# A routed two-layer product over 43 token tiles: hidden products made one tile ahead instead of two

## The chip, the core and the metric

The kernel runs on one core of a Trainium2 chip. The metric is device time in microseconds (us) for one execution. The engines are called as the profile calls them: PE (TensorE, with its weight loads as PEld), DVE (VectorE), ACT (ScalarE), POOL (GpSimd) and SP (SyncE).

## The reference

Three computations follow one another. The last of them, a mixture of experts with one expert for each token, is the part that this study is about.

```python
x = attention(q, k, v)                      # 8 x 576 tokens, 512 wide, linear attention
x = soft_mixture(x, phi, w1, w2)            # 32 slots; each token is a mixture of 32 slot outputs
# the last part, N = 4608 tokens, E = 8 experts, F = 1024
e_idx = np.argmax(x @ w_gate, axis=1)
gate_w = softmax(x @ w_gate)[arange(N), e_idx]
eom = 1 / (1 + exp(-(x @ w_output_gate)))
for e in range(E):
    mask = e_idx == e
    h = np.maximum(x[mask] @ w1[e], 0.0)
    out[mask] = gate_w[mask, None] * eom[mask, e, None] * (h @ w2[e])
```

## The kernel before

The first 318 us of the execution compute the attention, the slots, the gates, and a split of every expert's second weight into a high and a low float16 part (`w_pair`); the first weight is multiplied with the 32 slot outputs beforehand (`g_pair`). The tokens are sorted by expert into tiles of 128 rows. Room is made for `TILES` = 43 tiles, the most that 8 experts can need. In this execution tokens fill 36 of them, which PE's 864 long products (line 1773, 24 a tile) show; tiles 36 to 42 are empty.

Then comes the tile stage, a pipeline over the 43 tiles with two buffers of each kind (n = tile modulo 2):

- POOL **gathers** the sorted rows of a tile from a table in HBM by an indirect DMA (line 571), and later **stores** the result rows by an indirect DMA (line 578). Both stand in one queue; the order is written out by hand.
- DVE's `take` (line 1308) copies the gathered row into `c_rows`.
- PE's `turn` (line 1755) transposes it into bank 7, and DVE's `turn` (line 1312) copies it out to `c_stack`, counted by `cs_copied`. There is one such bank, so PE's next `turn` waits for DVE's last.
- PE's `hidden` (line 1761) makes 8 products of 128 columns into two banks, after reading the tile's expert number into a register (line 1759).
- ACT's `relu` (line 894, two halves) writes the high part `h_hi`; DVE's `low` (line 1318, two halves) writes the low part `h_lo`.
- PE's `second` (line 1773) makes 24 products of 512 columns into bank 4 + n, after another read of the expert number (line 1768). DVE's `finish` (line 1326) scales that into `y_out`, and POOL stores it.

PE makes `hidden` of tile t+2 just before `second` of tile t, in `step`. DVE's step t is turn(t+3), take(t+4), low(t+1), finish(t). From tile 36 on, PE runs `last_step`: it reads from `ended` whether tile t is empty, and if it is, skips both `hidden(t + 2)` and `second(t)`; two products of 2 by 2 (lines 1811 and 1813) stand in for them and raise the counts `y_done` and `h_done`. ACT, DVE and POOL run all 43 tiles in full; an empty tile's rows have row numbers out of bounds, so its gathers and stores move nothing.

## Time and profile before

| what | value |
|---|---|
| median of three executions | 567.01 us (564.3 to 567.61) |
| the profiled execution | 564.3 us, span 562.4 us |
| tile stage, from the first `take` to the last store's issue | 319.07 to 554.14 us |
| PE busy | 425.7 us, 76% of the span |
| DVE busy | 316.6 us, 56% |
| ACT busy, POOL busy | 222.4 us, 228.1 us |
| mean granted TensorE clock | 0.906 |

The clock is given as a share of 2.4 GHz; 0.50 is 1.2 GHz. The execution's own time is 1.9 us more than its span. Times inside the trace count from the span's start. A line number with a trailing "q" at its engine (PEldq, DVEq) is an instruction of that engine's sequencer, which reads the program and hands work to the engine.

### The profile page before, as it was taken

The numbers are of one execution on the slowest core, as the hardware profiler recorded it, in microseconds if no ns is written. First come the engines' busy times: TensorE is split into PE (matmuls) and PEld (weight loads), VectorE is DVE, ScalarE is ACT, GpSimd is POOL, SyncE is SP. The second block draws the span as 40 slices with busy tenths as digits, with TensorE's granted clock in tenths as the row PEclk, the third lists the DMA queues.
The fourth block names the chain that finished last, engine by engine and source line by source line (L and its number), as shares of the span: only waits on it lengthen the run. The fifth ranks groups of instructions, "written<-read, shape, count | busy, mean of one in ns | idle before, by whom it ended". The sixth has DMA issues, their size and how long they took to land.

```text
span 562.4 us, 12505 instructions
## 1 busy us (share of the span) xinstructions
PE 425.7 (76%) x4517; PEld 250.4 (45%) x4518; DVE 316.6 (56%) x491; ACT 222.4 (40%) x328; POOL 228.1 (41%) x145
## 2 busy tenths in 40 slices
PE   0468898888786627456677389999999999999910
PEld 0456676666454324352223144545454545454400
DVE  5999999994156460378396633434343433434372
ACT  0366676667313869484724211212121212121140
POOL 2255555553010487975500223333424242433342
PEclk9999999999769868677799679999999999999965
DMA  9769999956399999999595001111111111111100
GB/s 302 251 216 383 366 388 378 386 189 226 116 337 375 341 395 368 378 369 327 219 355 206 5 4 61 40 59 40 58 41 58 41 58 41 54 45 44 49 20 2
DMA packets 44855, 106.75 MB, mean 190 GB/s; under 512 B 4560, under 2 KB 5648, under 8 KB 44816
## 3 DMA queue, kind: packets, MB, share of 16 engines
q1 hardware_dynamic: 37888, 95.42, 46.1%
q0 software_dynamic: 4816, 10.06, 5.6%
q10 hardware_dynamic: 2112, 0.71, 0.6%
q8 instruction: 30, 0.49, 0.4%
q14 instruction: 9, 0.07, 0.0%
HBM read 96.25 MB, written 11.88 MB: 192 GB/s over the span
## 4 chain that ended last, share of the span: by engine, by line
PE 50%; DVE 16%; DMA 13%; ACT 7%; issue 6%; POOL 5%; SPq 0%; DVEq 0%; POOLq 0%; ACTq 0%
PE banks L1773 33%; DMA ring<-in_moe_w 6%; DMA big<-in_moe_w 4%; PE banks L1761 3%; DVE big L936 3%; POOL big L525 2%; DVE big L909 2%; PE banks L1638 2%; POOL big L554 2%; ACT big L712 2%; PE banks L1387 2%; DVE big L922 2%; PE banks L1558 1%; DVE big L928 1%; PE banks L1583 1%
## 5 line engine op out<-in xcount | busy, mean ns | idle before, releaser
L1773 PE MATMUL banks<-big,work 128*128 x864 | 193.8, 381 | 0.5 <-issue 0.5
L1773 PEld LDWEIGHTS banks<-big,work 128*128 128x128 f16 x864 | 83.4, 98 | 95.2 <-issue 2.5
L894 ACT ACTIVATE work<-banks 128x512 f16<-128x512 f32 x86 | 46.6, 595 | 185.7 <-PE banks L1773 170.4
L1326 DVE TENSOR_SCALAR work<-banks,tok,unscale 128x512 f32<-128x512 f32 x43 | 34.8, 809 | 130.2 <-PE banks L1773 124.9
L578 POOL DMA_INDIRECT out<-work,token_of x43 | 43.6, 1013 | 136.7 <-DVE split_ct L1308 124.4
L571 POOL DMA_INDIRECT tok<-token_rows,token_of x43 | 44.0, 1023 | 40.9 <-DVE token_of L1210 25.4
L525 POOL TENSOR_TENSOR big<-big 128x1152 f32<-128x1152 f32 x16 | 33.6, 2118 | 58.9 <-DVE big L941 58.9
L1318 DVE SCALAR_TENSOR_TENSOR work<-banks,work 128x512 f16<-128x512 f32 x86 | 55.0, 680 | 0.0
L1387 PE MATMUL banks<-big 64*64 64x128 f32 x1152 | 37.5, 283 | 7.5 <-ACT big L605 6.1
L1387 PEld LDWEIGHTS banks<-big 64*64 64x64 f32 x1152 | 33.8, 140 | 13.7 <-ACT big L605 11.7
L909 DVE TENSOR_REDUCE big<-big 128x256 f32<-128x2304 f32 x8 | 34.1, 4266 | 6.9 <-DMA big<-in_k 6.9
L518 POOL TENSOR_TENSOR big<-big 128x2304 f32<-128x2304 f32 x8 | 32.4, 4054 | 10.5 <-DVE big L928 10.4
L554 POOL TENSOR_TENSOR big<-big 128x2048 f16<-128x2048 f32 x8 | 32.6, 4079 | 8.7 <-ACT big L719 8.7
L554 POOL TENSOR_TENSOR big<-kvg,big 128x2048 f16<-128x2048 f32 x4 | 16.3, 4083 | 34.6 <-ACT kvg L719 34.6
L1761 PE MATMUL banks<-split_ct,kvg 128*128 128x128 f16 x304 | 24.9, 224 | 3.2 <-issue 1.9
L1638 PE MATMUL banks<-ring,split_ct 128*32 128x512 f32 x128 | 18.5, 704 | 10.4 <-ACT work L788 5.4
L1077 DVE TENSOR_REDUCE top_all<-banks 128x1 f32<-128x257 f32 (+1 forms) x16 | 5.7, 356 | 35.7 <-PE banks L1602 23.8
L605 ACT ACTIVATE big<-big 128x1152 f32<-128x1152 f32 x16 | 18.5, 1154 | 17.8 <-DVE big L922 17.7
L1421 PE MATMUL banks<-ident,big 128*128 128x128 f32 x144 | 21.9, 285 | 4.6 <-ACT kvg L663 3.7
L1558 PE MATMUL banks<-big,slot_in 128*32 128x256 f32 x192 | 15.6, 465 | 12.8 <-ACT side L730 7.2
L1072 DVE TENSOR_REDUCE top<-big 128x1 f32<-128x2048 f32 x8 | 18.1, 2276 | 9.3 <-DMA big<-in_moe_w 9.3
L1761 PEld LDWEIGHTS banks<-split_ct,kvg 128*128 x304 | 19.6, 98 | 8.4 <-issue 3.8
(219 smaller groups left out, 646.9 us busy)
## 6 DMA issues: line engine op xcount, KB each, us to landing
ring<-in_moe_w SPq DMA_DIRECT2D x12, 2048.0 KB, 10.2
big<-in_moe_w SPq DMA_DIRECT2D x10, 2048.0 KB, 11.6
big<-in_k SPq DMA_DIRECT2D x8, 1152.0 KB, 6.3
big<-in_q SPq DMA_DIRECT2D x8, 1152.0 KB, 7.0
big<-in_v SPq DMA_DIRECT2D x8, 1152.0 KB, 9.3
big<-in_moe_w SPq DMA_DIRECT2D x8, 1024.0 KB, 10.0
kvg<-in_moe_w SPq DMA_DIRECT2D x4, 1024.0 KB, 8.3
ring<-in_moe_w SPq DMA_DIRECT2D x4, 1024.0 KB, 10.7
```

What stands on the lines that cost most here:

```text
L518: pool.tensor_tensor(q_view(Q[b % 2]), q_view(Q[b % 2]), over_d(qtop[:, b % 2, :]), ALU.subtract).then_inc(q_shifted, 1)
L525: pool.tensor_tensor(q_view(QE[b % 3][:, part]), q_view(QE[b % 3][:, part]), over_d(qstat[:, b % 2, rec]), ALU.mult).then_inc(q_normed, 1)
L554: pool.tensor_tensor(lo, raw[:, u * HALF:(u + 1) * HALF], hi, ALU.subtract).then_inc(w_split, 1)
L571: pool.indirect_dma_start(out=srt[:, t, :], out_offset=None, in_=table, in_offset=bass.IndirectOffsetOnAxis(ap=token_of[:, t:t + 1].bitcas ...
L578: pool.indirect_dma_start(out=out, out_offset=bass.IndirectOffsetOnAxis(ap=token_of[:, t:t + 1].bitcast(U32), axis=0), in_=y_out[n], in_of ...
L894: act.activation(h_hi[n][:, b * 512:(b + 1) * 512], psum[2 * n + b], ACT.Relu).then_inc(h_hi_ready, 1)
L909: dve.tensor_reduce(out=kmax, in_=blocks(K[b % 2]).rearrange("p h (c d) -> p h d c", c=C), axis=X, op=ALU.max).then_inc(kmax_done, 1)
L1318: dve.scalar_tensor_tensor(h_lo[n][:, part], psum[2 * n + b], 0.0, h_hi[n][:, part], ALU.max, ALU.subtract).then_inc(h_lo_ready, 1)
L1326: dve.tensor_scalar(y_out[n], psum[4 + n], srt[:, ds(t, 1), NS], unscale[:, ds(ev, 1)], ALU.mult, ALU.mult).then_inc(y_scaled, 1)
L1387: last = pe.matmul(psum[a][64 * h:64 * h + 64, g * P:(g + 1) * P], blocks(K[b % 2])[r, 2 * g + h, c * D:(c + 1) * D], v_and_ones, start=c ...
L1761: i = pe.matmul(psum[2 * n + j // 4][:, j % 4 * P:(j % 4 + 1) * P], g_pair[:, ds(ev, 1), j * P:(j + 1) * P].rearrange("p o f -> p (o f)"), ...
L1773: last = pe.matmul(psum[4 + n], h[n][:, j * P:(j + 1) * P], w_pair[:, ds(ev, 1), w, j, :].rearrange("p o n -> p (o n)"), start=j == 0 and ...
```

## The change

The hidden products are made one tile ahead instead of two. PE's start-up loses one `turn` and one `hidden`; PE's step t becomes turn(t+2), hidden(t+1), second(t). DVE's step t becomes turn(t+2), take(t+3), low(t+1), finish(t). POOL starts with 5 gathers instead of 6, and gathers tile t+5 instead of t+6 after storing tile t. The separate `last_step` is gone: for the tiles from 36 on, `hidden(t+1)` is made whether or not a tile is empty, and only `second` stands under the condition. In `hidden` the read of the expert number stands before the wait for `cs_copied`. In `second` the waits for `h_hi` and `h_lo` are split: for the first half before product 0, for the second half before product 12. ACT's program is the same.

```diff
-            for t in range(2, 6):
+            for t in range(2, 5):
                 pool.wait_ge(c_rows_ready, t - 1)
                 gather(t)
             for t in range(TILES):
                 store(t, t % 2)
-                if t + 6 < TILES:
-                    pool.wait_ge(c_rows_ready, t + 5)
-                    gather(t + 6)
+                if t + 5 < TILES:
+                    pool.wait_ge(c_rows_ready, t + 4)
+                    gather(t + 5)
...
             take(2, 0, 32)
+            low(0, 0)
             turn(1, 1)
-            take(3, 1, 32)
-            low(0, 0)
-            turn(2, 0)
 
             def step(t, n, stored, count, static=None):
                 m = 1 - n
+                if static is None or static + 2 <= TILES - 1:
+                    turn(t + 2, n)
                 if static is None or static + 3 <= TILES - 1:
-                    turn(t + 3, m)
-                if static is None or static + 4 <= TILES - 1:
-                    take(t + 4, n, count)
+                    take(t + 3, m, count)
...
-            def hidden(t, n, early=True):
-
+            def hidden(t, n):
                 ev = pe.value_load(tile_e[0:1, ds(t, 1)], min_val=0, max_val=E - 1)
+                pe.wait_ge(cs_copied, t + 1)
...
-            def second(t, n, reused):
+            def second(t, n, reused, surely=True):
                 ev = pe.value_load(tile_e[0:1, ds(t, 1)], min_val=0, max_val=E - 1)
                 if reused:
                     pe.wait_ge(y_scaled, t - 1)
...
+                products_ = [(j, m) for j in range(FC) for m in range(3)]
+                if surely:
+                    for j, m in products_:
+                        if j % 4 == 0 and m == 0:
+                            pe.wait_ge(h_hi_ready, 2 * t + (j // 4 + 1))
+                            pe.wait_ge(h_lo_ready, 2 * t + (j // 4 + 1))
+                        last = products(j, m)
+                else:
+                    pe.wait_ge(h_hi_ready, 2 * t + 2)
+                    pe.wait_ge(h_lo_ready, 2 * t + 2)
+                    over = pe.value_load(ended[0:1, ds(t, 1)], min_val=0, max_val=E)
+                    with pe.If(over < E):
+                        for j, m in products_:
+                            products(j, m)
+
+                    last = pe.matmul(psum[6][0:2, 0:2], ones16[:, :], ones16[:, :], start=True, stop=True)
+                last.then_inc(y_done, 1)
...
-            hidden(1, 1)
-            turn(2, 0)
-
-            def step(t, n, static=None):
-                turn(t + 3, 1 - n)
-                pe.wait_ge(cs_copied, t + 3)
-                pe.wait_ge(h_hi_ready, 2 * t + 2)
-                pe.wait_ge(h_lo_ready, 2 * t + 2)
-                hidden(t + 2, n)
-                second(t, n, static is None).then_inc(y_done, 1)
...
+            def step(t, n, static=None, surely=True):
+                if static is None or static + 2 <= TILES - 1:
+                    turn(t + 2, n)
+                if static is None or static + 1 <= TILES - 1:
+                    hidden(t + 1, 1 - n)
+                second(t, n, static != 0 and static != 1, surely)
```

On DVE, at the start of the tile stage (`split_ct<-tok` is take, `split_ct<-banks` is turn, `work<-banks,work` is low), the two programs differ so:

```order
 L1312 COPY split_ct<-banks 128x128 [waits cs_done]
 L1308 COPY split_ct<-tok 128x128 [waits gathered0]
-L1312 COPY split_ct<-banks 128x128 [waits cs_done]
+L1318 SCALAR_TENSOR_TENSOR work<-banks,work 128x512 [waits h_hi_ready] x2
+L1312 COPY split_ct<-banks 128x128 [waits cs_done] x2
 L1308 COPY split_ct<-tok 128x128 [waits gathered1]
 L1318 SCALAR_TENSOR_TENSOR work<-banks,work 128x512 [waits h_hi_ready] x2
-L1312 COPY split_ct<-banks 128x128 [waits cs_done] x2
```

The first `low` stands one `turn` and one `take` earlier, ahead of the `take` of tile 3.

On PE, at the head of a step in the loop, the program before has the end of `second`, then `turn`, then `hidden` (`banks<-split_ct,kvg`):

```order
619 L1773 MATMUL banks<-big,work 128x512 x2
620 L1752 REGISTER_ALU
621 L1755 MATMUL banks<-ident,split_ct 128x128 [waits cs_copied,c_rows_ready]
622 L1792 ISA [waits cs_copied]
623 L1759 ISA [waits h_lo_ready,h_hi_ready]
624 L1759 TENSOR_LOAD tile_e
625 L1759 ISA x2
626 L1761 ISA
627 L1761 MATMUL banks<-split_ct,kvg 128x128
```

The waits for `h_lo` and `h_hi` stood ahead of the read of the expert number and of `hidden`.

The changed program has there, on PE:

```order
601 L1772 MATMUL banks<-big,work 128x512 x2
602 L1750 REGISTER_ALU
603 L1753 MATMUL banks<-ident,split_ct 128x128 [waits cs_copied,c_rows_ready]
604 L1756 ISA
605 L1756 TENSOR_LOAD tile_e
606 L1756 ISA x2
607 L1759 ISA [waits cs_copied]
608 L1759 MATMUL banks<-split_ct,kvg 128x128
```

Only the wait for `cs_copied` is left ahead of `hidden`, and it stands behind the read.

The waits for `h_lo` and `h_hi` now stand ahead of `second` on PE:

```order
622 L1759 MATMUL banks<-split_ct,kvg 128x128
623 L1766 TENSOR_LOAD tile_e
624 L1766 ISA x2
625 L1780 ISA [waits y_scaled]
626 L1772 ISA [waits h_lo_ready,h_hi_ready]
627 L1772 MATMUL banks<-big,work 128x512
```

They moved past `hidden` and past the second read of the expert number.

In a step of the tiles from 36 on, PE had this before (`<-side` is the read of `ended`):

```order
682 L1755 MATMUL banks<-ident,split_ct 128x128 [waits cs_copied]
683 L1804 ISA [waits cs_copied]
684 L1806 ISA [waits h_lo_ready,h_hi_ready]
685 L1806 TENSOR_LOAD side
686 L1806 ISA x2
687 L1807 COMPARE_AND_BRANCH
688 L1759 ISA
```

The branch stood ahead of `hidden`, so an empty tile cost one read.

The changed program has there, behind its 8 `hidden` products:

```order
684 L1766 ISA
685 L1766 TENSOR_LOAD tile_e
686 L1766 ISA x2
687 L1768 REGISTER_ALU
688 L1784 ISA [waits y_scaled]
689 L1786 REGISTER_ALU [waits h_lo_ready,h_hi_ready]
690 L1786 TENSOR_LOAD side
691 L1786 ISA x2
692 L1787 COMPARE_AND_BRANCH
```

The branch stands behind `hidden` and behind a read of the expert number.

On POOL, at the last stores and gathers of the program (`tok<-` is a gather, `out<-` a store):

```order
 L578 DMA out<-work,token_of 4608x512 [waits y_scaled]
 L571 DMA tok<-token_rows,token_of 128x33 [waits c_rows_ready]
-L578 DMA out<-work,token_of 4608x512 [waits y_scaled] x6
+L578 DMA out<-work,token_of 4608x512 [waits y_scaled]
+L571 DMA tok<-token_rows,token_of 128x33 [waits c_rows_ready]
+L578 DMA out<-work,token_of 4608x512 [waits y_scaled] x5
 L51 UNCONDITIONAL_BRANCH
```

The last gather stands behind one more store.

## Rows read from the trace of the kernel before

**Rows 1.** The chain that ended last, in order of time: start us, us, what.

```profile
327.99 6.80 PE banks L1773 x24
...
340.53 0.45 PE banks L1761 x8
340.98 5.18 PE banks L1773 x24
346.21 0.45 PE banks L1761 x8
```

**Rows 2.** Busy time of each engine in the middle stretch, granted clock, DMA.

```profile
340.00:530.00 190.00, 190.00 (x1109) 95.46 (x1107) 75.61 (x170) 36.90 (x68) 67.43 (x67) 1.00 0.15 48
```

**Rows 3.** PE's sequencer, 340.5 to 346.2: operation, ns min/median/max, first and last start us.

```profile
L1793 PEldq EVENT_SEMAPHORE  x1: 51/51/51, 342.9 to 342.9; - x1
...
L1759 PEldq TENSOR_LOAD <-tile_e x1: 300/300/300, 343.1 to 343.1; - x1
...
L1768 PEldq TENSOR_LOAD <-tile_e x1: 300/300/300, 344.9 to 344.9; - x1
L1768 PEldq SEQ_ASSERT  x1: 18/18/18, 345.6 to 345.6; - x1
```

**Rows 4.** Timeline, one step: start us, us, engine, line, operation [idle before].

```profile
341.58 1.28 DVE L1318 SCALAR_TENSOR_TENSOR work<-banks,work 128x512 f16<-128x512 f32 x2
```

**Rows 5.** Timeline of the first tiles.

```profile
322.48 0.20 DVE L1308 COPY split_ct<-tok 128x128 f16<-128x128 f16 x1 [2.54 <-DMA tok<-token_rows,token_of]
...
323.85 1.28 DVE L1318 SCALAR_TENSOR_TENSOR work<-banks,work 128x512 f16<-128x512 f32 x2
...
325.05 0.21 DVE L1312 COPY split_ct<-banks 128x128 f16<-128x128 f16 x1
...
326.28 1.19 PE L1761 MATMUL banks<-split_ct,kvg 128*128 128x128 f16 x8 [0.61 <-issue]
...
327.99 6.80 PE L1773 MATMUL banks<-big,work 128*128 x24 [0.52 <-issue]
```

**Rows 6.** PE's sequencer before the first long product, 325 to 328.2.

```profile
L1754 PEldq EVENT_SEMAPHORE  x1: 51/51/51, 325.3 to 325.3; - x1
...
L1768 PEldq TENSOR_LOAD <-tile_e x1: 306/306/306, 327.2 to 327.2; - x1
```

**Rows 7.** Half a microsecond in which the clock rises: us, PE busy, PEclk.

```profile
330.50:331.00 0.50, 0.50 (x3) 0.54 0.00 0
```

**Rows 8.** Timeline of the empty tiles.

```profile
536.84 1.02 POOL L571 DMA_INDIRECT tok<-token_rows,token_of  x1 [0.31 <-issue]
...
538.17 1.02 POOL L578 DMA_INDIRECT out<-work,token_of  x1 [0.30 <-issue]
539.49 1.02 POOL L571 DMA_INDIRECT tok<-token_rows,token_of  x1 [0.31 <-issue]
540.37 0.20 DVE L1308 COPY split_ct<-tok 128x128 f16 x1 [3.42 <-DMA tok<-token_rows,token_of]
...
540.70 0.29 PE L1755 MATMUL banks<-ident,split_ct 128*128 128x128 f16 x1 [3.10 <-DVE split_ct L1308]
...
542.56 0.18 DVE L1308 COPY split_ct<-tok 128x128 f16<-128x128 f16 x1
...
543.34 1.02 POOL L578 DMA_INDIRECT out<-work,token_of  x1 [2.82 <-DVE work L1326]
...
544.70 1.28 DVE L1318 SCALAR_TENSOR_TENSOR work<-banks,work 128x512 f16<-128x512 f32 x2
...
547.05 0.16 PE L1811 MATMUL banks<-ones 128*2 128x2 f16 x1 [1.73 <-ACT work L894]
...
549.41 0.98 POOL L578 DMA_INDIRECT out<-work,token_of  x1 [0.93 <-DVE work L1326]
...
552.53 0.81 DVE L1326 TENSOR_SCALAR work<-banks,tok,unscale 128x512 f32<-128x512 f32 x1 [1.95 <-DMA out<-work,token_of]
554.14 0.98 POOL L578 DMA_INDIRECT out<-work,token_of  x1 [1.77 <-DVE work L1326]
```

More of the change, by code:

```diff
@@ L1346, in step @@
                 finish(t, n, stored)
-            step(0, 0, None, 48, 0)
+            step(0, 0, None, 32, 0)
             step(1, 1, None, 48, 1)
-            with dve.Fori(1, (TILES - 5) // 2) as h:
-                step(2 * h, 0, h, 16 * h + 48)
+            with dve.Fori(1, (TILES - 5) // 2 + 1) as h:
+                step(2 * h, 0, h, 16 * h + 32)
                 step(2 * h + 1, 1, h, 16 * h + 48)
-            for t in range(TILES - 5, TILES):
-                step(t, t % 2, t // 2, 16 * ((t + 4) // 2 + 1), t)
+            for t in range(TILES - 3, TILES):
+                step(t, t % 2, t // 2, 16 * ((t + 3) // 2 + 1), t)
         @block.tensor
@@ L1770, in second, with products @@
                     pe.wait_ge(y_scaled, t - 1)
-                for j in range(FC):
-                    for m, (h, w) in enumerate(((h_hi, 0), (h_hi, 1), (h_lo, 0))):
-                        last = pe.matmul(psum[4 + n], h[n][:, j * P:(j + 1) * P],
-                                         w_pair[:, ds(ev, 1), w, j, :].rearrange("p o n -> p (o n)"),
-                                         start=j == 0 and m == 0, stop=j == FC - 1 and m == 2)
-                return last
+                def products(j, m):
+                    h, w = ((h_hi, 0), (h_hi, 1), (h_lo, 0))[m]
+                    return pe.matmul(psum[4 + n], h[n][:, j * P:(j + 1) * P],
+                                     w_pair[:, ds(ev, 1), w, j, :].rearrange("p o n -> p (o n)"),
+                                     start=j == 0 and m == 0, stop=j == FC - 1 and m == 2)
+                products_ = [(j, m) for j in range(FC) for m in range(3)]
[14 more added lines that the diff above has]
+                last.then_inc(y_done, 1)
             pe.wait_ge(g_split, E)
@@ L1781, in _ @@
             turn(0, 0, False)
-            pe.wait_ge(cs_copied, 1)
             hidden(0, 0)
             turn(1, 1)
-            pe.wait_ge(cs_copied, 2)
-            hidden(1, 1)
-            turn(2, 0)
-            def step(t, n, static=None):
-                turn(t + 3, 1 - n)
-                pe.wait_ge(cs_copied, t + 3)
-                pe.wait_ge(h_hi_ready, 2 * t + 2)
-                pe.wait_ge(h_lo_ready, 2 * t + 2)
-                hidden(t + 2, n)
-                second(t, n, static is None).then_inc(y_done, 1)
-            def last_step(t, n, static=None):
-                if static is None or static + 3 <= TILES - 1:
-                    turn(t + 3, 1 - n)
-                follows = static is None or static + 2 <= TILES - 1
-                if follows:
-                    pe.wait_ge(cs_copied, t + 3)
-                pe.wait_ge(h_hi_ready, 2 * t + 2)
-                pe.wait_ge(h_lo_ready, 2 * t + 2)
-                over = pe.value_load(ended[0:1, ds(t, 1)], min_val=0, max_val=E)
-                with pe.If(over < E):
-                    if follows:
-                        hidden(t + 2, n, False)
-                    second(t, n, True)
-                pe.matmul(psum[6][0:2, 0:2], ones16[:, :], ones16[:, :], start=True, stop=True).then_inc(y_done, 1)
-                if follows:
-                    pe.matmul(psum[6][0:2, 0:2], ones16[:, :], ones16[:, :], start=True, stop=True).then_inc(h_done, 2)
+            def step(t, n, static=None, surely=True):
[4 more added lines that the diff above has]
+                second(t, n, static != 0 and static != 1, surely)
             step(0, 0, 0)
```

8 lines of the change are left out of this document (4 added, 4 removed).

## The prediction

> **What bounds the kernel now.** I read the chain that ended last first, because the change touches one stage only and the page's shares are averages over many. The reader is to see in it a step of 5.68 us: hidden products start at 340.53 us and again at 346.21, 0.45 us of them, then 24 long products of 5.18 us, and nothing between [rows 1]. The row by stretches says the same: PE is busy 190.00 of 190.00 us at a granted clock of 1.00 [rows 2]. So in tiles 1 to 35 PE's array is the bound, and a change of order can win nothing there; it can only open gaps. The stage has two ends where PE is not full, the start (until the first long product at 327.99 us) and the empty tiles (from about 533.6 us: 327.99 + 6.80 + 35 x 5.68). There other waits end last, and there the change is decided. Next I read PE's sequencer rows, which tell how far the sequencer runs ahead of the array, and the two timelines.
>
> **Full tiles: nothing.** The products per tile are the same, and between the first long product and the last the array still has 35 groups of hidden products. DVE's turn, take, low and finish keep their order, and gather t+5 behind store t is taken in DVE's step t+2, as gather t+6 was. What is new is cover: hidden(t+1) comes 5 us before its tile's second, not 11 us. But relu waited until the buffer's last user, second(t-1), was done in both programs, so it starts only the 0.45 us of the hidden products later. Low runs from 341.58 to 342.86 [rows 4]; allow 0.5 us, 343.4. The long products that need it start about 346.66 on the array. Cover is left: 3.3 us. The sequencer comes earlier. Before, it stood at the wait for low until 342.9, read the expert number at 343.1, again at 344.9, and was past that read at 345.6 [rows 3], 1 us before the array wanted the long products. With the wait moved behind the hidden products, it passes from turn straight to the read, some 0.6 us sooner, and finds low done. The four added or moved semaphore waits cost about 0.05 us each (the duration of such an instruction in rows 3) on a sequencer that is 1 us ahead: I take 0. The bounds: below, 0, since the array has no gap to give; above, four fully exposed ones, 0.2 us a step, 7 us in 35.
>
> **The start: a gain of 1.2 us.** Before, the first long product hung on take(3) and turn(2): low(0) at 323.85, the copy of tile 2 at 325.05, hidden products at 326.28, long ones at 327.99 [rows 5]. Now low(0) stands right behind take(2), which started at 322.48 and takes 0.20 us; low(0) begins at 322.68 and the copy of tile 1 follows it after the same 1.20 us, at 323.88 instead of 325.05. PE has the same to do behind it: turn, read, 8 hidden products, read, long products. In the trace that took 327.99 - 325.05 = 2.94 us, so the first long product starts at 326.8, 1.2 us earlier. hidden(0) may start 0.3 to 0.5 us sooner by its earlier read; low(0) waits for the gather of tile 2 anyway, so this is covered. What the clock does with the 1.2 us is a bound. It rose from 1.2 to 2.4 GHz near 330.95 [rows 7], some 3 us into the first group, which took 6.80 us instead of 5.18. If it rises with the work, all 1.2 us stay. If it rises at the same instant, the 1.2 us are run at half speed and 0.6 stay. If it rises clearly sooner, up to 1.6 us more come (the whole excess of 6.80 over 5.18). I take 1.2, since the pattern of work ahead of it is the same but for one group of eight products.
>
> Here a page speaks. In the row, the sequencer stood at the wait for `cs_copied` of line 1754 until 325.3, just after the copy ended, and only then went on to its read [rows 6]. The Trainium skill, "Perfetto Trace Analysis", section "Sequencer Loop", has it that an engine instruction is pushed into a queue and waits for its semaphores there, so the sequencer goes on. By that rule the read would be done while turn waits, and the start would gain 2.0 us, not 1.2. The row shows the wait as an instruction of the sequencer's own, so I keep 1.2 and price the other below as a rival.
>
> **The empty tiles: a loss of 4.6 us.** Two prices change.
>
> First, the gather. Before, tile 42 was gathered behind store(36), at 539.49, and taken at 542.56 without a wait; that is 3.07 us at most. The gather at 536.84, behind a store with real data, was taken at 540.37, 3.53 us later. Now tile 42 is gathered behind store(37), which starts at 543.34; a gather follows a store by 1.32 us (538.17 to 539.49), so at 544.66, and take(42) comes at 547.7 (548.2 by the other row). Before, DVE had begun low(40) at 544.70 [rows 8]. That alone is 3.1 us.
>
> Second, PE's sequencer. An empty tile before cost turn, one read of `ended`, a branch and two tiny products: low ended at 544.70 + 1.28 = 545.98 and the tiny product started at 547.05, 1.07 us [rows 8]. Now each empty tile up to 41 has a read of the expert number, 8 hidden products, a second read, and only then that 1.07. A read until its first product is 327.99 - 327.2 = 0.79 us [rows 5, 6]; the pushing of 8 products is 327.2 - 326.28 = 0.92. So 0.79 + 0.92 + 0.79 + 1.07 = 3.57 us a step, where a step took some 2.0 us before. Followed through:
> - take(40) is still released at 540.37 by the gather behind store(35), and PE's turn at 540.70; the tiny product of step 38 starts at 544.3, of step 39 at 547.9.
> - turn(42) needs take(42) at 547.7 plus 0.33, so 548.0: the two prices meet here, and do not add. Step 40 ends at 551.6, step 41 at 555.2.
> - step 42 has no hidden products: 0.79 + 1.07, so 557.1. DVE's last finish follows at once; before it was at 552.53.
> - its other condition, the output buffer: finish(40) 551.7, its store 1.61 us behind (552.53 to 554.14), free 3.12 us after that (549.41 to 552.53), so 556.4. Not the later one.
>
> The loss is 557.1 - 552.5 = 4.6 us. What follows the last finish, the store at 554.14 and the end of the program, only shifts. Finish(37) is not moved, since PE's step 37 ends near 538.5 (533.6, some 1.3 us for DVE's finish and take, and 3.57), and DVE comes to it at 541.7 after the late gather. Bounds: 3.1 if only the gather counts and DVE keeps its old pace; 5.9 if the gather takes 3.53 and the hidden products at the low clock (1.19 us instead of 0.92, [rows 5]) are exposed three times.
>
> **Sum.** 0 - 1.2 + 4.6 = +3.4 us. On the profiled execution that is 564.3 to 567.7. That one is the fastest of the three runs; the median, 567.01, is 2.7 us above it, and the same sum on it gives **570.4 us**.
>
> **Rivals.**
> - *The program does more than is written for the start* (the sequencer does go on past a waiting turn). Then hidden products follow the copy's end, 324.1, by 0.2 us, and the long ones follow at 324.3 + 0.92 + 0.79 = 326.0. A gain of 2.0, so 569.6. For it: an earlier read is what the edit in `hidden` makes possible. Against it: rows 6. Chance 0.10.
> - *The tail is covered.* The reads overlap with the waits, the gather of empty rows lands within 0.5 us, and only the start counts: 565.8. Against it: the take at 540.37 waited 3.42 us for a gather of empty rows. Chance 0.07.
> - *Slower by more than 1%: the full tiles open a gap.* The place is the head of `second`: if the sequencer is not ahead when it comes to the moved waits, the reads and waits show on the array, as they did at the start, where the array stood 0.61 us ahead of the hidden and 0.52 us ahead of the long products [rows 5]. Four exposed waits give +7, so 577; both gaps whole would give 1.13 x 35 = 40 us, 610. It decides from (5.7 - 3.4) / 35 = 0.07 us a step. Against it: the lead of 1 us in rows 3, which grows. Chance 0.08, nearly all at the small end.
> - *The clock stays low through the first tile*, since one group of hidden products less precedes it. The 17 long products after the rise would cost 0.21 us more each, +3.6, so 574. Chance 0.05.
> - *Faster by more than 1%* needs a shorter step, and the array has none to give, so a tail shorter than before. Chance 0.02.
>
> **How the numbers follow.** My forecast has the remaining 0.68, with its own range from 567 to 573. A measurement of this kernel can tell about 1% (5.7 us) from no change. Slower by over 1%: the two slow rivals, 0.13, and the upper end of my tail, 0.04, so 0.17. Faster: 0.02. Same: 0.81. Range: the sum's lowest is 3.1 - 2.8 = +0.3 and its highest 5.9 - 0.6 = +5.3, so 567.3 to 572.3; the runs shown lie 0.6 above and 2.7 below their median, and the covered tail at 565.8 lies just under it. I take 566.0 to 573.3.
>
> **What would show it.** The step stays 5.68 us and PE busy 190 of 190 in the middle. The first long product starts at 326.8. The take of the last tile waits about 3 us for its gather. The tiny products of the last tiles lie 3.6 us apart instead of 2, and the last finish is 4.6 us later with respect to the end of the last long product. It is wrong if gaps stand ahead of the first or the thirteenth long product of a tile, or if the first group takes far more than 6.8 us.

## The result, and the profile after

The changed kernel takes 569.84 us (median, 566.71 to 571.44) against 565.91 us (564.3 to 567.8) of the kernel before in the same series, 14 runs each: a ratio of 1.0062, with a 95% interval of 1.0043 to 1.0083. It is slower by 3.9 us, less than 1%. Its profiled execution took 569.95 us, its span is 568.2 us.

The two profiled executions differ by 5.8 us in their spans, but 2.0 us of that lie ahead of the changed stage: the first take starts at 321.04 us instead of 319.07, in code that the change does not touch. From here on the stage is measured from its own marks: the first take, the first long product, and DVE's finish of tiles 0, 35 and 42 (all from the timelines).

| stretch, us | before | after | difference |
|---|---|---|---|
| first take to first long product | 8.92 | 7.67 | -1.25 |
| first long product to finish(0) | 6.95 | 7.68 | +0.73 |
| finish(0) to finish(35), 35 full tiles | 198.93 | 198.93 | 0.00 |
| finish(35) to finish(42), the empty tiles | 18.66 | 22.97 | +4.31 |
| sum | 233.46 | 237.25 | +3.79 |

**The full tiles.** The chain that ended last in the changed kernel, in order of time (start us, us, what; line 1772 is the long products, 1759 the hidden ones):

```profile
341.97 0.45 PE banks L1759 x8
342.42 5.18 PE banks L1772 x24
...
347.65 0.45 PE banks L1759 x8
```

The period is 347.65 - 341.97 = 5.68 us, as in [rows 1], and the row by stretches (us, PE, PEld, DVE, ACT, POOL, clock, DMA) has PE full, as in [rows 2]:

```profile
340.00:530.00 190.00, 190.00 (x1109) 95.46 (x1108) 74.25 (x166) 35.99 (x67) 67.91 (x67) 1.00 0.15 49
```

PE's sequencer in one of these steps (ns min/median/max, first and last start us). The long products of this step start at 342.42:

```profile
L1756 PEldq TENSOR_LOAD <-tile_e x1: 303/303/303, 338.3 to 338.3; - x1
...
L1766 PEldq TENSOR_LOAD <-tile_e x1: 305/305/305, 340.1 to 340.1; - x1
L1766 PEldq SEQ_ASSERT  x1: 18/18/18, 340.7 to 340.7; - x1
```

The read for the hidden products is at 338.3 and the read for the long ones over at 340.7, 1.7 us ahead of the array, where it was 1 us before [rows 3]. Low for the next tile is done early too:

```profile
343.02 1.28 DVE L1318 SCALAR_TENSOR_TENSOR work<-banks,work 128x512 f16<-128x512 f32 x2
```

It ends at 344.30, and the long products that need it start at 347.65 + 0.45 = 348.10, so 3.8 us of cover are left in this step.

**The start.** The timeline of the changed kernel, to be held against [rows 5]:

```profile
324.46 0.20 DVE L1308 COPY split_ct<-tok 128x128 f16<-128x128 f16 x1 [2.55 <-DMA tok<-token_rows,token_of]
324.57 1.28 DVE L1318 SCALAR_TENSOR_TENSOR work<-banks,work 128x512 f16<-128x512 f32 x2
...
325.77 0.22 DVE L1312 COPY split_ct<-banks 128x128 f16<-128x128 f16 x1
...
326.91 1.16 PE L1759 MATMUL banks<-split_ct,kvg 128*128 128x128 f16 x8 [0.51 <-DVE split_ct L1312]
...
328.71 7.53 PE L1772 MATMUL banks<-big,work 128*128 x24 [0.64 <-ACT work L894]
```

low(0) follows take(2) directly, and the first long product starts 4.25 us after take(2) instead of 5.51. From the copy of tile 1 (325.77) to the first long product it is 2.94 us, as it was from the copy of tile 2 before. But its group takes 7.53 us, where it took 6.80. Half microseconds of the same stretch (us, PE busy, PEclk, DMA share, GB/s):

```profile
330.50:331.00 0.50, 0.50 (x3) 0.50 0.00 0
...
333.00:333.50 0.50, 0.50 (x4) 0.85 0.00 0
```

The clock is still 0.50 (1.2 GHz) at 331 and rises to 2.4 GHz within the row at 333.0, some 4.4 us after the first long product; before it was 3 us after [rows 7]. That takes 0.7 of the 1.25 us back. Counted from the first take, the rise comes after 12.1 us here and after 11.9 us before: work that started earlier did not bring it forward.

**The empty tiles.** The timeline of the changed kernel, to be held against [rows 8] (line 1791 is the tiny product, 1308 take, 571 the gather, 1326 finish):

```profile
540.28 0.16 PE L1791 MATMUL banks<-ones 128*2 128x2 f16 x1 [1.76 <-issue]
540.60 0.20 DVE L1308 COPY split_ct<-tok 128x128 f16 x1 [2.14 <-DMA tok<-token_rows,token_of]
...
543.51 0.20 DVE L1308 COPY split_ct<-tok 128x128 f16 x1 [0.64 <-DMA tok<-token_rows,token_of]
...
544.91 1.02 POOL L571 DMA_INDIRECT tok<-token_rows,token_of  x1 [0.31 <-issue]
...
544.97 0.16 PE L1791 MATMUL banks<-ones 128*2 128x2 f16 x1 [1.88 <-DVE work L1318]
...
547.23 0.20 DVE L1308 COPY split_ct<-tok 128x128 f16 x1 [0.95 <-DMA tok<-token_rows,token_of]
...
548.95 0.16 PE L1791 MATMUL banks<-ones 128*2 128x2 f16 x1 [1.65 <-DVE work L1318]
...
552.78 0.16 PE L1791 MATMUL banks<-ones 128*2 128x2 f16 x1 [1.47 <-DVE work L1318]
...
556.19 0.17 PE L1791 MATMUL banks<-ones 128*2 128x2 f16 x1 [1.44 <-DVE work L1318]
...
557.98 0.16 PE L1791 MATMUL banks<-ones 128*2 128x2 f16 x1 [1.63 <-DVE work L1326]
...
558.29 0.81 DVE L1326 TENSOR_SCALAR work<-banks,tok,unscale 128x512 f32<-128x512 f32 x1 [0.98 <-PE banks L1791]
```

The tiny products lie 4.69, 3.98, 3.83, 3.41 and 1.79 us apart. Tile 42 is taken at 547.23, 2.32 us after its gather was issued and after 0.95 us of waiting; the next tiny product, at 548.95, is not late by it. So in this run it is not the gathers that set the pace. Nor is it low. Low of tile 40 and the sequencer's wait for it (line 1785, in `second` of tile 40, whose tiny product is the one at 552.78):

```profile
547.55 1.29 DVE L1318 SCALAR_TENSOR_TENSOR work<-banks,work 128x512 f16<-128x512 f32 x2
```

```profile
L1785 PEldq EVENT_SEMAPHORE  x1: 51/51/51, 551.7 to 551.7; - x1
```

Low ends at 548.84, and the sequencer comes to the wait 2.9 us later.

The take that the gather behind store(35) releases came 2.32 us after that gather here (538.28 to 540.60) and 3.53 us after it in the kernel before (536.84 to 540.37, [rows 8]). The table of DMA queues for the time of that gather in the kernel before, 536.84 to 540.24 (packets, MB, share of 16 engines), has a row that the same table of the changed kernel, for 538.28 to 540.47, does not have:

```profile
q8 instruction: 1, 0.02, 2.0%
```

It is one transfer on the queue for instructions. It starts at 538.12 in the kernel before, 1.3 us behind the gather, and at 540.99 in the changed one, when the gather has landed. In both it starts 0.7 us after the tiny product of tile 37. PE comes to that product later in the changed kernel, and so the transfer does not meet the gather. The section on the hardware has the other traces.

### The profile page after: what moved, and what is told of

It reads as the page before. It is cut to its first block, busy times and chain, and to the rows that moved or that the text cites. A ratio compares the mean times of both kernels' runs of the same rounds, so it can differ in the third digit from the quotient of the medians.

```text
span 568.2 us, 12744 instructions
## 1 busy us (share of the span) xinstructions
PE 436.2 (77%) x4552; PEld 255.2 (45%) x4553; DVE 317.4 (56%) x491; ACT 222.8 (39%) x328; POOL 228.5 (40%) x145
## 4 chain that ended last, share of the span: by engine, by line
PE 53%; DVE 16%; DMA 9%; ACT 9%; issue 6%; POOL 5%; DVEq 0%; POOLq 0%; SPq 0%; ACTq 0%
PE banks L1772 33%; DMA big<-in_moe_w 4%; PE banks L1759 3%; PE banks L1385 2%; DVE big L936 2%; POOL big L525 2%; DVE big L909 2%; POOL big L554 2%; DMA ring<-in_moe_w 2%; ACT big L712 2%; PE banks L1419 2%; PE banks L1556 1%; PE banks L1636 1%; PE banks L1581 1%; PE banks L1463 1%
## 5 line engine op out<-in xcount | busy, mean ns | idle before, releaser
L1759 PE MATMUL banks<-split_ct,kvg 128*128 128x128 f16 x344 | 30.4, 229 | 4.3 <-issue 3.0
L1759 PEld LDWEIGHTS banks<-split_ct,kvg 128*128 x344 | 23.4, 99 | 11.0 <-issue 5.4
L1636 PE MATMUL banks<-ring,split_ct 128*32 128x512 f32 x128 | 20.5, 770 | 9.1 <-DMA ring<-in_moe_w 5.7
L605 ACT ACTIVATE big<-big 128x1152 f32<-128x1152 f32 x16 | 18.5, 1154 | 17.7 <-DVE big L922 17.6
L663 ACT ACTIVATE kvg<-banks 128x512 f32<-128x512 f32 (+1 forms) x40 | 20.5, 553 | 6.8 <-PE banks L1419 6.6
```

The source lines that it names most:

```text
L1759: i = pe.matmul(psum[2 * n + j // 4][:, j % 4 * P:(j % 4 + 1) * P], g_pair[:, ds(ev, 1), j * P:(j + 1) * P].rearrange("p o f -> p (o f)"), ...
```

## The experiments

Twelve kernels were run (e6 and e7 with two executions each, e9 with four, the others with 6 to 12). For each the marks of its profiled execution stand in this table: first take to first long product, finish(0) to finish(35) divided by 35, finish(35) to finish(42), and first take to finish(35). The times are medians; the ratio is against the kernel before in the same series.

| run | start | full tile | empty tiles | take to finish(35) | median | ratio (95%) |
|---|---|---|---|---|---|---|
| before | 8.92 | 5.684 | 18.66 | 214.80 | 565.91 | |
| after | 7.67 | 5.684 | 22.97 | 214.28 | 569.84 | 1.0062 (1.0043 to 1.0083) |
| e1_skip | 7.63 | 5.684 | 22.87 | 213.89 | 570.23 | 1.0078 (1.0055 to 1.0102) |
| e2_gather6 | 7.67 | 5.684 | 22.96 | 214.47 | 570.20 | 1.0077 (1.0053 to 1.0102) |
| e3_both | 7.63 | 5.683 | 20.56 | 214.03 | 567.98 | 1.0028 (1.0007 to 1.0049) |
| e4_read_in_if | 7.49 | 5.684 | 20.22 | 213.83 | 566.45 | 1.0012 (0.9989 to 1.0035) |
| e5_ended_first | 7.62 | 5.684 | 17.92 | 213.97 | 564.41 | 0.9978 (0.9960 to 0.9995) |
| e6_after_low3 | 10.41 | 5.684 | 29.99 | 216.81 | 579.18 | 1.0231 (1.0197 to 1.0265) |
| e7_before_low3 | 11.61 | 6.630 | 29.75 | 251.07 | 612.79 | 1.0824 (1.0791 to 1.0858) |
| e8_before_start | 8.86 | 5.697 | 18.79 | 214.98 | 564.88 | 0.9992 (0.9974 to 1.0010) |
| e9_waits8 | 7.67 | 5.991 | 23.76 | 224.51 | 580.28 | 1.0244 (1.0220 to 1.0268) |
| e10_gather_first | 8.95 | 5.684 | 16.21 | 214.41 | 563.62 | 0.9960 (0.9942 to 0.9978) |
| e11_gather_first_start | 8.80 | 5.684 | 16.16 | 214.62 | 563.84 | 0.9958 (0.9938 to 0.9977) |
| e12_ended_gather_first | 7.67 | 5.683 | 17.51 | 213.96 | 564.87 | 0.9964 (0.9940 to 0.9987) |

The 5.697 of e8 comes from one late tile: the finishes of tiles 3 and 4 lie 6.13 us apart instead of 5.68. Its gather of tile 7 took 4.5 us from its issue (345.65) to the take (350.18), and a transfer of instructions starts at 348.06.

### What the loss in the empty tiles is made of

**e1_skip.** The changed kernel, with an empty tile skipped by PE as before (for the tiles from 36 on; the full ones are as in the changed kernel, and `second_plain` is the 24 long products):

```diff
                 if static is None or static + 2 <= TILES - 1:
                     turn(t + 2, n)
-                if static is None or static + 1 <= TILES - 1:
-                    hidden(t + 1, 1 - n)
-                second(t, n, static != 0 and static != 1, surely)
...
+                if follows:
+                    pe.wait_ge(cs_copied, t + 2)
+                pe.wait_ge(h_hi_ready, 2 * t + 2)
+                pe.wait_ge(h_lo_ready, 2 * t + 2)
+                over = pe.value_load(ended[0:1, ds(t, 1)], min_val=0, max_val=E)
+                with pe.If(over < E):
+                    if follows:
+                        hidden(t + 1, 1 - n, False)
+                    second_plain(t, n)
+                pe.matmul(psum[6][0:2, 0:2], ones16[:, :], ones16[:, :], start=True, stop=True).then_inc(y_done, 1)
+                if follows:
+                    pe.matmul(psum[6][0:2, 0:2], ones16[:, :], ones16[:, :], start=True, stop=True).then_inc(h_done, 2)
```

> The changed program, but for tiles 36 to 42 PE skips the hidden products and the reads of the expert number where tile t is empty, as the kernel before did; hidden stays one tile ahead. Theory A (PE's sequencer sets the pace of the empty tiles): tiny products return from 3.4-4.7 us apart to some 2 us, first finish of an empty tile to last finish gets about 3 us shorter than in the changed kernel, total about 566.6 (before + 0.7, the rest being the gather of tile 42 behind store(37)). Theory B (the gather distance sets it): the tail stays 3 us or more longer than before and the total near 569.5.

Nothing was won: 22.87 us, 570.2. Theory A missed; theory B's numbers (3 us or more longer than before, near 569.5) came, but e2, next, takes the gather distance away as their cause in the changed kernel, and the timeline shows another one (1820 is the tiny product):

```profile
537.57 1.02 POOL L571 DMA_INDIRECT tok<-token_rows,token_of  x1 [0.31 <-issue]
...
541.31 0.19 DVE L1308 COPY split_ct<-tok 128x128 f16 x1 [3.61 <-DMA tok<-token_rows,token_of]
...
547.31 0.16 PE L1820 MATMUL banks<-ones 128*2 128x2 f16 x1 [2.82 <-DVE split_ct L1312]
...
550.62 0.16 PE L1820 MATMUL banks<-ones 128*2 128x2 f16 x1 [2.10 <-issue]
...
550.86 1.09 ACT L894 ACTIVATE work<-banks 128x512 f16<-128x512 f32 x2 [2.15 <-PE banks L1822]
...
551.49 1.29 DVE L1318 SCALAR_TENSOR_TENSOR work<-banks,work 128x512 f16<-128x512 f32 x2 [0.85 <-ACT work L894]
...
553.84 0.17 PE L1820 MATMUL banks<-ones 128*2 128x2 f16 x1 [3.03 <-issue]
```

Two things are seen. Tile 40 is taken 3.74 us after its gather, where the changed kernel had it after 2.32; that is 1.4 us more. As in the kernel before, PE skips the work of an empty tile and comes to the tiny product of tile 37 early (538.15), and the transfer of instructions (538.85) meets the gather. And the tiny products, though only one read and a branch each, are still 3.2 to 3.3 us apart. Between two of them stand relu (550.86, ready only when the tiny product at 550.62 had raised `h_done`), then low (551.49 to 552.78), then 1.06 us of wait, read and branch until 553.84. That is a closed loop: the tiny product that raises `h_done` (line 1822) stands behind the wait for low. With two tiles ahead the tiny product of step t raised `h_done` for tile t+2, so relu and low of that tile had a whole further step; with one tile ahead it raises it for tile t+1, and step t+1 waits for it. The changed kernel itself does not have this loop, since its hidden products stand ahead of the wait for low.

**e2_gather6.** The changed kernel, with POOL's distance of before:

```diff
-            for t in range(2, 5):
+            for t in range(2, 6):
...
-                if t + 5 < TILES:
-                    pool.wait_ge(c_rows_ready, t + 4)
-                    gather(t + 5)
+                if t + 6 < TILES:
+                    pool.wait_ge(c_rows_ready, t + 5)
+                    gather(t + 6)
```

> The changed program with POOL's distance of before: 6 gathers ahead, gather t+6 behind store t. Theory A: PE's sequencer still sets the pace, so the waits of the last takes for their gathers vanish, and the time falls by 0 to 0.7 us only, about 569.4. Theory B: the tail shrinks by about 3 us, total about 566.5.

The empty tiles take 22.96 us (22.97 in the changed kernel), and the median is 570.2. The distance alone costs nothing here; theory B falls as the cause of the loss in the changed kernel.

**e3_both.** Both edits together.

> Both edits: empty tiles skipped by PE and the gather distance of before. Both theories: the tail is that of before (18.7 us from finish(35) to finish(42)) within 0.3 us, and what is left is the start: first take to the first long product 1.2 us shorter than before, of which the clock may take back up to 0.7. Total 565.3 (before - 0.6).

20.56 us instead of the 18.7 that both theories gave, and 568.0 us. It is 2.3 us better than e1 by the marks, so the gathers do matter once PE is quicker; but with PE's work and POOL's order of before, 1.9 us stay. Only the loop just told is left to explain them, as the tiny products are 3.3 us apart here too.

**e4_read_in_if.** The changed kernel with its hidden products for empty tiles, but without one of its reads:

```diff
             def second(t, n, reused, surely=True):
-                ev = pe.value_load(tile_e[0:1, ds(t, 1)], min_val=0, max_val=E - 1)
+                if surely:
+                    ev = pe.value_load(tile_e[0:1, ds(t, 1)], min_val=0, max_val=E - 1)
...
                     with pe.If(over < E):
+                        ev = pe.value_load(tile_e[0:1, ds(t, 1)], min_val=0, max_val=E - 1)
```

> The changed program with the read of the expert number of the long products moved behind the branch, so an empty tile does one read less (0.79 us on PE's sequencer) but still its hidden products. Theory A: 0.79 us less for each of steps 38 to 42, of which the output buffers take back one: 3 us less than the changed kernel, about 566.8. Theory B: no change, about 569.8.

It came out as theory A had it: 2.75 us less in the empty tiles, 566.45 us (566.8 was expected). Three of its tiny products:

```profile
545.25 0.16 PE L1793 MATMUL banks<-ones 128*2 128x2 f16 x1 [1.00 <-ACT work L894]
...
548.38 0.16 PE L1793 MATMUL banks<-ones 128*2 128x2 f16 x1 [0.78 <-ACT work L894]
...
551.13 0.16 PE L1793 MATMUL banks<-ones 128*2 128x2 f16 x1 [0.75 <-ACT work L894]
```

Each of the five steps that lost the read and still make hidden products is 0.4 to 0.7 us shorter than in the changed kernel, a little less than the 0.79 us from a read to its first product. So the changed kernel is bound by PE's sequencer there. The second of the two distances shown is 2.75 us (548.38 to 551.13), below the 3.3 us of the loop in e1: that loop does not hold the changed kernel, not even with less work for the sequencer.

**e5_ended_first.** e3_both with the read of `ended` moved out of the loop:

```diff
+                over = pe.value_load(ended[0:1, ds(t, 1)], min_val=0, max_val=E)
                 pe.wait_ge(cs_copied, t + 2)
                 pe.wait_ge(h_hi_ready, 2 * t + 2)
                 pe.wait_ge(h_lo_ready, 2 * t + 2)
-                over = pe.value_load(ended[0:1, ds(t, 1)], min_val=0, max_val=E)
                 with pe.If(over < E):
```

> The kernel with both edits (empty tiles skipped, gather distance of before), where PE reads whether the tile is empty before it waits for low, not behind. Theory C: with hidden one tile ahead the empty tiles form a loop, tiny product, relu, low, wait, read, branch, tiny product, of 3.3 us, where two tiles ahead it went round only every second tile. The read then leaves the loop: the tiny products lie some 2.5 us apart instead of 3.3, finish(35) to finish(42) falls from 20.6 to 17.5-18.5 us, the time from 568.0 to about 565.5. Theory A (PE's sequencer alone, each read counts): the read is only moved, the pace stays 3.3 us, 568.0.

Its timeline, one turn of the loop:

```profile
546.49 0.16 PE L1820 MATMUL banks<-ones 128*2 128x2 f16 x1 [1.77 <-DVE work L1318]
...
546.73 1.09 ACT L894 ACTIVATE work<-banks 128x512 f16<-128x512 f32 x2 [1.49 <-PE banks L1822]
...
547.36 1.29 DVE L1318 SCALAR_TENSOR_TENSOR work<-banks,work 128x512 f16<-128x512 f32 x2 [0.18 <-ACT work L894]
...
549.05 0.16 PE L1820 MATMUL banks<-ones 128*2 128x2 f16 x1 [2.37 <-DVE work L1318]
```

The tiny products are 2.56 us apart instead of 3.3, with the same instructions on every engine. The empty tiles take 17.92 us and the median is 564.41, as theory C had it (2.5 us, 17.5 to 18.5, 565.5). The loop is shown: the same read costs 0.7 us a tile inside it and nothing outside. A version that skips empty tiles but raises `h_done` ahead of the wait for low was not run.

### The full tiles: how much cover is left

**e6_after_low3 and e7_before_low3.** In both kernels every half of low is made three times, the extra ones into an unused place of `tok` (their results are not used):

```diff
+                    for k in (0, 1):
+                        dve.wait_ge(extra_done, 4 * t + (2 * b + k))
+                        dve.scalar_tensor_tensor(extra, psum[2 * n + b], 0.0, h_hi[n][:, part],
+                                                 ALU.max, ALU.subtract).then_inc(extra_done, 1)
                     dve.scalar_tensor_tensor(h_lo[n][:, part], psum[2 * n + b], 0.0, h_hi[n][:, part],
                                             ALU.max, ALU.subtract).then_inc(h_lo_ready, 1)
```

> The changed kernel with every half of low made three times (the two extra ones into an unused place), 2.6 us and more of work added between relu and the long products. It measures the cover. By my prediction 3.3 us of cover are left in a full tile, and the wait for low stands behind the hidden products and the reads, so a full tile stays near 5.68 us, or gets up to 0.5 us longer if the extra waits between the copies of low eat the rest; the time rises by 10 us at most in the full tiles and some 15 in the empty ones. If one tile ahead leaves no cover, each full tile gets the whole 2.6 us: +90 us.

> The kernel before with the same threefold low. Its wait for low stands ahead of both reads and the hidden products, 1.7 us of sequencer work. If the place of the wait matters: low ends 2.6 us or more later, at about 345.5-346 in the step that begins at 340.5, the long products cannot follow before 347.5-348, so each full tile gets 1 to 1.5 us longer, some 35 to 50 us in all, more than the changed kernel with the same edit. If two tiles ahead gives the better cover, it rises by less than the changed kernel.

The middle stretch of the changed kernel with this edit (us, PE, PEld, DVE, ACT, POOL, clock, DMA share, GB/s):

```profile
340.00:530.00 190.00, 190.00 (x1102) 95.21 (x1101) 161.32 (x301) 35.83 (x66) 68.60 (x68) 1.00 0.15 50
```

The same stretch of the kernel before with this edit, and below it who PE waited for (line 1780 is the long products, 1768 the hidden ones):

```profile
340.00:530.00 190.00, 174.50 (x947) 86.75 (x945) 138.32 (x259) 31.38 (x58) 58.62 (x58) 1.00 0.13 42
```

```profile
PE banks L1780 <- issue: 10.5, 14, 0.8
PE banks L1768 <- issue: 5.0, 14, 0.4
```

With DVE more than twice as busy, the changed kernel keeps PE full and its tile at 5.684 us; the kernel before loses 0.95 us a tile, with gaps of up to 0.8 us ahead of the long products, put down to issue (no engine but PE's own sequencer ends them), in 14 of some 29 tiles. The step on cover is borne out as far as it was tried: some 2.6 us of it were used here without a gap. The reason is seen in the kernel before: its sequencer has both reads and the hidden products still to do after low's end. The two kernels differ in more than the place of this wait, though, and no run moved the wait alone. In this respect the change makes the full tiles more robust. At low's real length neither kernel needs it.

**e9_waits8.** The changed kernel with a pair of waits ahead of each of the 8 groups of a tile's long products:

```diff
-                        if j % 4 == 0 and m == 0:
+                        if m == 0:
```

> The changed kernel with the pair of waits for h_hi and h_lo ahead of every product group (8 pairs a tile instead of 2), all already met. If a met wait costs the array nothing while the sequencer is ahead (my step): the full tile stays 5.68 us, time as the changed kernel, 569.8. If waits in the middle of the long products cost 0.05 us each on the array: 12 more of them give 0.6 us a tile, +21 us.

Neither expectation: 5.991 us a tile, +0.31, where 0 or 0.6 was expected. Who PE waited for in the middle stretch (total us, times, longest):

```profile
PE banks L1772 <- DVE work L1326: 3.5, 7, 0.5
PE banks L1772 <- ACT work L894: 3.2, 7, 0.5
```

The gaps are half a microsecond, ahead of the long products, in 14 of some 32 tiles, and not one at each wait. Twelve more waits, all for things long done, cost 0.31 us in all, 0.026 each. It fits a sequencer that is ahead by a certain stock, which a few waits don't exhaust (the changed kernel's own split costs nothing) and twelve more do; how much of its time a met wait takes was not measured by itself.

### The start

**e8_before_start.** The kernel before, with DVE's order of the changed one at the start:

```diff
             turn(1, 1)
-            take(3, 1, 32)
             low(0, 0)
+            take(3, 1, 32)
             turn(2, 0)
```

> The kernel before with DVE's low(0) moved ahead of take(3), nothing else: the start part of the change alone. If the gain at the start comes from DVE's order: first take to the first long product 8.9 -> 7.9 to 8.0 us, the rest as before, time 0.4 to 1.0 us less than before. If it comes from PE's shorter start (one turn and one group of hidden products less): unchanged, 8.9.

8.86 us: no gain. Its timeline:

```profile
325.14 1.27 DVE L1318 SCALAR_TENSOR_TENSOR work<-banks,work 128x512 f16<-128x512 f32 x2
...
326.02 1.17 PE L1761 MATMUL banks<-split_ct,kvg 128*128 128x128 f16 x8 [1.43 <-DVE split_ct L1312]
...
327.03 0.26 PE L1755 MATMUL banks<-ident,split_ct 128*128 128x128 f16 x1
...
327.33 0.22 DVE L1312 COPY split_ct<-banks 128x128 f16<-128x128 f16 x1 [0.82 <-PE banks L1755]
```

low(0) is at 325.14, more than a microsecond earlier with respect to take(2) than in [rows 5], and the copy of tile 2 (327.33) does not follow it. It waits for PE's turn at 327.03, and that stands behind the hidden products of tile 1 at 326.02. So the start was held by PE's own order as much as by low(0), and the change gains there only because PE also makes one group of hidden products less ahead of the first long one. The reverse, PE's shorter start with DVE's old order, was not run.

### Versions that are faster than both

**e10_gather_first.** The kernel before, with POOL's gather ahead of its store:

```diff
             for t in range(TILES):
-                store(t, t % 2)
                 if t + 6 < TILES:
                     pool.wait_ge(c_rows_ready, t + 5)
                     gather(t + 6)
+                store(t, t % 2)
```

> The kernel before with POOL's order in a step swapped: gather(t+6) ahead of store(t). If the 3.4 us wait of take(41) before is the gather standing behind store(35): the gather starts near finish(35) + 1.1 us, take(41) comes 2 to 3 us sooner, and the time falls by 2 to 3 us. If the tail is set by the stores and the output buffers (one more issue of 1.3 us ahead of each store): no gain, or up to 1.3 us more.

The timeline: the gather of tile 41 at 532.17 stands ahead of store(35) at 536.53, tile 41 is taken at 537.89 without a wait (3.42 us of waiting in [rows 8]), and finish(37) comes at 539.54.

```profile
532.17 1.02 POOL L571 DMA_INDIRECT tok<-token_rows,token_of  x1 [0.31 <-issue]
...
536.53 1.02 POOL L578 DMA_INDIRECT out<-work,token_of  x1 [3.34 <-DVE split_ct L1308]
...
537.89 0.18 DVE L1308 COPY split_ct<-tok 128x128 f16 x1
...
539.54 0.81 DVE L1326 TENSOR_SCALAR work<-banks,tok,unscale 128x512 f32<-128x512 f32 x1 [0.27 <-DMA out<-work,token_of]
```

The empty tiles take 16.21 us instead of 18.66, and the time is 563.62 us, a ratio of 0.9960 (0.9942 to 0.9978), as the first of the two expectations had it.

**e11_gather_first_start.** e10 with the edit of e8.

> The two edits of the runs on the kernel before together (low(0) ahead of take(3), gather ahead of store). If both gains are real they add, since one lies at the start and one at the end: 2.5 to 4 us less than before, about 563. If the start's gain is taken back by the clock, as the time of the gather edit alone.

563.84 us, 16.16 us in the empty tiles: the gather edit's gain and nothing more, as e8 makes one expect.

**e12_ended_gather_first.** e5_ended_first with gather(t+5) ahead of store(t), where e5 has gather(t+6) behind it; so POOL's distance differs as well as its order.

> The changed kernel with hidden one tile ahead, empty tiles skipped, the read of `ended` ahead of the waits, and POOL's gather(t+5) ahead of store(t). If the loop of the empty tiles (2.5 us each) and the gathers are what is left there: finish(35) to finish(42) 16.0 to 17.0 us (17.9 without the gather edit), and with the shorter start about 563.0, below both kernels. If the wait for the output buffer of store(35), 1.5 us in the run without the gather edit, stays: 17.5 to 18, and 564.4 as there.

17.51 us and 564.87 us, in a series in which the kernel before had 566.82: a ratio of 0.9964. This is the second of the two expectations: finish(37) still waits for the output buffer of store(35), as this row of its timeline shows:

```profile
542.34 0.81 DVE L1326 TENSOR_SCALAR work<-banks,tok,unscale 128x512 f32<-128x512 f32 x1 [1.09 <-DMA out<-work,token_of]
```

The three versions e10, e11 and e12 cannot be told apart; each is 0.4% faster than the kernel before and, by the two ratios, about 1% faster than the changed one (0.996 / 1.0062 = 0.990). e5, without the gather edit, lies just behind them (0.9978, 0.9960 to 0.9995).

## Why the prediction was right, and where its steps were not

The time forecast was 570.4 us and the measured one is 569.84; the forecast difference was +3.4 us and the measured one +3.9 by the medians, +3.8 by the marks. The forecast time stood on a median of three executions, 567.01 us, which is 1.1 us above the 565.91 of fourteen; a part of its closeness is luck.

- **Full tiles, 0.** Right, to the hundredth (198.93 us for 35 tiles in both). The reason given, a sequencer that is ahead and 3.3 us of cover, was tried by e6 and e9; the rows show 3.8 us of cover. A threefold low opened no gap in the changed kernel (e6). The slow rival shows only with many more waits (e9, 12 more a tile, +0.31 us).
- **The start, -1.2.** The size was right (-1.25), and so was the chain in the changed kernel: low(0) right behind take(2), the copy of tile 1 after the same 1.20 us, the long products 2.94 us behind it. What the step did not say is that moving low(0) gains nothing by itself: e8 shows that as long as PE makes one more group of hidden products first, the copy waits for PE's turn. Two chains ended at the same place, and I named one.
- **The clock at the start.** The term was mis-sized: I kept all 1.2 us, and in the profiled execution 0.73 went back, since the clock rose 4.4 us after the first long product instead of 3. Of the cases that the prediction named, the one that came is its lower bound, a rise at the same instant, with 0.6 kept: in the eight traces with this start and low's real length the clock rises 11.1 to 12.5 us after the first take, in the four with the old start 11.1 to 11.9. 0.52 us were kept in the profiled execution, just under that bound. Over the seven of these kernels with the same full tile, first take to finish(35) is 0.3 to 1.0 us shorter than before, 0.7 in the mean. The sign that the prediction gave for being wrong, a first group of far more than 6.8 us, came in part (7.53).
- **The rival on the waiting `turn`** (gain 2.0) did not come: 1.25 was measured, in line with the row of [rows 6] that the sequencer itself stood at the wait. The Trainium skill's rule ("Perfetto Trace Analysis", "Sequencer Loop") is about waits that an engine instruction carries. The wait here was an instruction of the sequencer's own, and no run here tries the rule.
- **The empty tiles, +4.6.** +4.31 measured. That PE's sequencer sets the pace, by the reads and the hidden products, is shown by e4 (one read less, -2.75 us). The size is right partly by luck, by misses that nearly cancel. The take behind store(35)'s gather came 5.28 us after finish(35) (535.32 to 540.60), where the forecast had 6.50 (533.87 to 540.37): 1.2 us less, by a gather that landed sooner. The transfer of instructions no longer met it, which the forecast did not foresee. From PE's turn behind that take to the last tiny product it was 17.0 us (540.96 to 557.98) instead of 16.4: the distances are 4.69, 3.98, 3.83 and 3.41 where the forecast had 3.57 each. And the last finish stands 0.3 us behind the last tiny product, which I had put at nothing.
- **The gather of the last tile** was priced too high: its take came 2.32 us after it, not 3.07, and waited 0.95 us where I had about 3 as a sign. By e2 POOL's distance costs nothing in the changed kernel. I had said that the two prices meet and do not add; they do not, and the sequencer's came out the later.
- **What my expectations of e1 and e3 did not see** is the loop through relu and low that one tile ahead closes when an empty tile is skipped in the manner of before. It is no part of the changed kernel's time.

## What to carry to other kernels

In a software pipeline with work that may be empty, look at the empty iterations by themselves: an engine that is full otherwise hides a long way round through three engines, and in the skipping versions here (e1, e3) only there did the number of tiles ahead become a period. A read into a register cost 0.8 us of the sequencer here, and 1.1 with the branch on it; put them ahead of the wait whose end they would otherwise lengthen, and behind the branch if only one side needs them. Where a gather and a store share a queue, try the one that someone waits for first: in the kernel before this was worth 2.45 us of the empty tiles (e10), in e12 only 0.4.

## What the runs showed of the hardware

- From the issue of a gather of 128 rows directly behind the store of the last full tile to the take that waited for it, it took 2.32 us in the changed kernel (538.28 to 540.60), 2.31 in e4 (536.04 to 538.35) and 2.31 in e9, but 3.53 us in the kernel before, 3.74 in e1 and 3.81 in e8. What goes with it is one transfer on the queue for instructions (q8). It starts 0.7 us after the tiny product of tile 37 in twelve of the fourteen traces, and 0.95 and 1.2 us after it in e12 and e9. In the seven traces in which a gather of an empty tile took over 3 us to land (before, e1, e8, e9, e10, e11, e12) this transfer starts 0.8 to 1.4 us after that gather's issue. In these seven the landing takes 3.1 to 3.7 us. In the 227 gathers of the tile stage whose landing is on record and behind which no such transfer starts within 0.1 to 2.2 us, it takes 2.2 to 2.6 us. That the transfer holds the gather up is inferred from this; no run moved it by itself. The store next to it behaves alike: finish(37) waited for it until 541.19 in e5 (store issued at 536.29, 4.9 us) and until 539.54 in e10 (536.53, 3.0 us); the transfer of instructions starts 1.9 us after that store in e5 and 2.6 us after it in e10.
- Of waits on PE's sequencer for things long done, the two more that the changed kernel has in a full tile cost the array nothing (5.684 us in both), and 12 further ones cost 0.31 us a tile (e9). That a lead is used up in between is my reading and was not measured.
- With one group of hidden products fewer ahead of them, the long products began earlier and ran 4.4 instead of 3 us at 1.2 GHz in the profiled execution, so half of what an earlier start gained was lost at the lower clock. Over the traces with low's real length it is 3.4 to 4.8 us with the new start and 2.1 to 3.0 with the old one.
